# Routing per chunk inside the recurrence, a region of rows per expert, and tokens kept in expert order

## The chip, the cores and the metric

The kernel runs on one core of a Trainium2 chip. Times are device microseconds (us) of one execution. The core has five engines that run side by side, each with its own instruction stream: PE (TensorE, matrix products, with its weight loads as PEld), DVE (VectorE), ACT (ScalarE), POOL (GpSimd) and SP (SyncE, which issues transfers here). They are kept in step by semaphores that instructions raise and wait for. Transfers (DMA) can be issued by SP, ACT and POOL; an indirect one, whose rows go to addresses held in a tile, by POOL.

## What is computed

A delta-rule recurrence over 768 tokens for 4 sequences of 8 heads (head size 48), then a top-1 mixture of 8 experts, then a dense mixture of 4 experts whose shares are an input:

```python
for t in range(S):                                   # recurrence
    y[:, :, t] = q_t @ state
    state = state + bt * outer(k_t, v_t - state @ k_t)
# x = y as [3072 tokens, 384]
logits = x @ w_gate;  e_idx = argmax(logits, axis=1)  # MoE1, 8 experts, F = 1024
out[mask] = gate_w * sigmoid(x @ w_output_gate)[e] * (relu(x[mask] @ w1[e]) @ w2[e])
p = domain_probs / (domain_probs.sum(-1) + 1e-9)      # MoE2, 4 experts, F = 1024
out = sum_e p[:, e:e+1] * (relu(x @ w1[e]) @ w2[e])
```

## The kernel before, in words

**Recurrence** (to about 340 us). The 768 steps are cut into 12 chunks (NC) of 64. Each chunk needs the inverse of a triangular matrix per head, which is made in levels: DVE substitutes the small blocks (`substitute`, L1083/L1086), and PE and DVE join them over two levels; DVE turns the half-made inverse with the transpose of L1123 into X (X32), and PE multiplies with it in `level32_left` (L525). The work of chunks c+1 to c+4 is interleaved by hand in one loop over c on every engine. A chunk gives two tiles of 128 tokens (NP = 2, in all NT = 24): ACT copies them from PSUM to `x_all` (L890), PE turns them and multiplies with the gate weights, and ACT copies the logits of the chunk (L907). SP zeroes a DRAM buffer `x_sorted` (33 x 192 KB) in the meantime (`clear`).

**Routing** (340 to 390 us). With all logits there, DVE finds each token's expert (L1235 to L1241), PE sums ones below each token (its rank) and over each tile, and DVE makes of them the position of every token in an order by expert (L1246 to L1262), each expert starting at a multiple of 128 rows. POOL scatters the 24 tiles by one indirect DMA each (L480) into `x_sorted`. DVE makes a table of which expert a slot of 128 rows belongs to (`slot_i`), then the gate scale and the shares of each token. The weights of expert 0 are loaded, rounded by ACT (L986) and their low parts taken by DVE (L1298).

**MoE1** (390 to 700 us). Every product is made as three products of high and low parts (`three`: L735, L736, L737). A loop over 31 slots of 128 rows; in one pass PE does `up(s)`, turns the next tile (`tokens_turned`, L742), `down(s - 1)` and turns the hidden rows (L766). DVE takes the relu, the turned tiles (L1308, L1310) and hidden rows (L1323, L1325), and copies the result to `y_sb` (L1329). SP loads a tile ahead (`load_tile`) and writes `y_sb` to `y_sorted`. PE and ACT read a slot's expert from `slot_i` by register loads (L746, L749). POOL takes the low parts of the next expert's weights.

**Between the layers** (700 to 717 us). POOL gathers every token's row back from `y_sorted` (L501), ACT scales it (L995), PE turns it, ACT and DVE take high and low part, and POOL, ACT and DVE prepare the first half expert of MoE2.

**MoE2** (from 717 us). 4 experts in 2 halves each, over 8 blocks of 384 tokens: 64 steps of the same length. DVE adds each result, times its share, to `acc`, which is the storage of `x_all` (L1372). SP writes the tiles out (L440).

## Time and profile before

| | us |
|---|---|
| median of 3 executions | 1530.92 (1529.55 to 1543.22) |
| profiled execution, device time | 1532.9 |
| its span, first to last instruction | 1531.1 |
| PE busy | 1421.6 (93% of the span) |
| DVE busy | 664.8 (43%) |
| ACT busy | 289.8 (19%) |
| POOL busy | 256.1 (17%) |
| mean granted clock of PE | 0.96 of full speed |

Shares of busy time are averages over all stages. The granted clock is 1.00 at 2.4 GHz and 0.50 at 1.2 GHz; a stretch between shows that both occurred in it. The device time of an execution is a little above its span.

### The profile page before, as it was taken

The numbers are of one execution on the slowest core, as the hardware profiler recorded it, in microseconds if no ns is written. First come the engines' busy times: TensorE is split into PE (matmuls) and PEld (weight loads), VectorE is DVE, ScalarE is ACT, GpSimd is POOL, SyncE is SP. The second block draws the span as 40 slices with busy tenths as digits, with TensorE's granted clock in tenths as the row PEclk, the third lists the DMA queues.
The fourth block names the chain that finished last, engine by engine and source line by source line (L and its number), as shares of the span: only waits on it lengthen the run. The fifth ranks groups of instructions, "written<-read, shape, count | busy, mean of one in ns | idle before, by whom it ended". The sixth has DMA issues, their size and how long they took to land.

```text
span 1531.1 us, 36843 instructions
## 1 busy us (share of the span) xinstructions
PE 1421.6 (93%) x14814; PEld 1370.9 (90%) x14815; DVE 664.8 (43%) x1301; ACT 289.8 (19%) x631; POOL 256.1 (17%) x132
## 2 busy tenths in 40 slices
PE   5799999980799999995999999999999999999998
PEld 5799999970688888995999999999999999999998
DVE  5567676624455555553443333333333333333332
ACT  2223323122011121002331111111111111111111
POOL 1001011006533343202232002020020020200000
PEclk7899999985899999997999999999999999999999
DMA  6455454216333333114121001000010010000122
GB/s 135 99 123 125 110 119 101 73 47 249 129 113 128 123 123 121 42 42 145 47 68 42 0 0 41 0 13 28 0 41 0 0 41 0 0 0 0 28 50 46
DMA packets 106538, 99.27 MB, mean 65 GB/s; under 512 B 58128, under 2 KB 95376, under 8 KB 106448
## 3 DMA queue, kind: packets, MB, share of 16 engines
q1 hardware_dynamic: 88176, 61.81, 15.6%
q10 hardware_dynamic: 15200, 26.68, 5.4%
q0 software_dynamic: 3072, 9.44, 1.8%
q8 instruction: 75, 1.23, 0.3%
q14 instruction: 15, 0.12, 0.0%
HBM read 72.72 MB, written 25.17 MB: 64 GB/s over the span
## 4 chain that ended last, share of the span: by engine, by line
PE 84%; DMA 5%; SPq 3%; DVE 2%; POOL 2%; issue 2%; ACT 1%; ACTq 0%; DVEq 0%
PE bank L735 23%; PE bank L737 23%; PE bank L736 23%; PE bank L525 8%; DMA kq_sb<-in_kq_dram 2%; POOL x_sorted L480 2%; PE bank L766 2%; SPq L328 1%; DMA inverse_blocks<-inverse 1%; PE bank L640 1%; PE bank L643 1%; PE bank L659 1%; SPq L310 1%; PE bank L742 1%; ACT R L862 1%
## 5 line engine op out<-in xcount | busy, mean ns | idle before, releaser
L735 PE MATMUL bank<-x2Th,v1h 128*128 (+1 forms) x768 | 257.3, 335 | 3.6 <-issue 3.6
L1363 DVE SCALAR_TENSOR_TENSOR gTl<-bank,gTh 128x384 fp32r<-128x384 f32 x256 | 142.7, 557 | 269.9 <-ACT gTh L1006 269.9
L735 PE MATMUL bank<-v2h,gTh 128*128 128x384 f32 x768 | 258.3, 336 | 0.0
L737 PE MATMUL bank<-x2Th,v1l 128*128 (+1 forms) x768 | 257.1, 335 | 0.0
L736 PE MATMUL bank<-x2Tl,v1h 128*128 (+1 forms) x768 | 257.1, 335 | 0.0
L737 PE MATMUL bank<-v2h,gTl 128*128 128x384 f32 x768 | 256.6, 334 | 0.0
L736 PE MATMUL bank<-v2l,gTh 128*128 128x384 f32 x768 | 256.6, 334 | 0.0
L1006 ACT ACTIVATE gTh<-bank 128x384 fp32r<-128x384 f32 x256 | 126.0, 492 | 637.2 <-PE bank L737 637.2
L1372 DVE SCALAR_TENSOR_TENSOR x_all<-bank,p_sb,x_all 128x384 f32 (+1 forms) x192 | 106.7, 611 | 258.9 <-PE bank L737 258.9
L735 PEld LDWEIGHTS bank<-x2Th,v1h 128*128 128x128 f32 x768 | 144.7, 188 | 4.0 <-issue 4.0
L736 PEld LDWEIGHTS bank<-x2Tl,v1h 128*128 128x128 f32 x768 | 144.8, 188 | 0.0
L737 PEld LDWEIGHTS bank<-x2Th,v1l 128*128 128x128 f32 x768 | 144.6, 188 | 0.0
L736 PEld LDWEIGHTS bank<-v2l,gTh 128*128 128x128 f32 x768 | 144.3, 188 | 0.0
L735 PEld LDWEIGHTS bank<-v2h,gTh 128*128 128x128 f32 x768 | 144.3, 188 | 0.0
L737 PEld LDWEIGHTS bank<-v2h,gTl 128*128 128x128 f32 x768 | 144.2, 188 | 0.0
L510 POOL CAST v1h<-v_raw 128x1536 fp32r<-128x1536 f32 x7 | 10.3, 1473 | 478.2 <-PE bank L737 478.2
L735 PE MATMUL bank<-w2h,hTh 128*128 x248 | 86.3, 348 | 2.5 <-DVE hTl L1325 2.5
L737 PE MATMUL bank<-w2h,hTl 128*128 x248 | 84.1, 339 | 0.0
L736 PE MATMUL bank<-w2l,hTh 128*128 x248 | 83.9, 338 | 0.0
L735 PE MATMUL bank<-w1h,xsTh 128*128 x186 | 76.9, 413 | 7.5 <-issue 4.8
L525 PE MATMUL bank<-kq_sb 64*64 64x64 f32 (+1 forms) x1536 | 60.0, 233 | 16.6 <-ACT R L862 7.6
L737 PE MATMUL bank<-w1h,xsTl 128*128 x186 | 74.1, 398 | 0.0
(167 smaller groups left out, 1920.8 us busy)
## 6 DMA issues: line engine op xcount, KB each, us to landing
w_raw<-in_moe_w_dram ACTq DMA_DIRECT2D x16, 1536.0 KB, 7.0
v_raw<-in_moe_w_dram SPq DMA_DIRECT2D x16, 768.0 KB, 4.5
x_sorted<-zeros SPq DMA_DIRECT2D x33, 192.0 KB, 3.8
xs_in<-x_sorted SPq DMA_DIRECT2D x33, 192.0 KB, 2.3
y_sorted<-y_sb SPq DMA_DIRECT2D x31, 192.0 KB, 1.9
kq_sb<-in_kq_dram SPq DMA_DIRECT2D x28, 192.0 KB, 3.8
kt_sb<-in_kt_dram SPq DMA_DIRECT2D x24, 196.0 KB, 3.4
vt_sb<-in_vt_dram SPq DMA_DIRECT2D x24, 192.0 KB, 4.3
```

Source lines behind the costliest of these rows:

```text
L310: sp.dma_start(gram_blocks[n % 2, u].rearrange("h j i -> j h i"), R[rows, n % NR, :, cols])\
L328: sp.dma_start(Y[rows, n % NY, :, cols], inverse_blocks[n % 2, u].rearrange("h j i -> j h i"))\
L480: pool.indirect_dma_start(out=x_sorted, out_offset=bass.IndirectOffsetOnAxis(ap=pos[:, t:t + 1], axis=0), in_=x_all[:, t, :], in_offset=No ...
L525: return pe.matmul(dst, lhsT, rhs, start=True, stop=True)
L640: pe.matmul(bank[5 + p][half_rows(a), small(p, h)], kq_sb[half_rows(a), c % NKQ, 1, h], state[half_rows(a), c % 2, h], start=True, stop=False)
L735: pe.matmul(dst, lh, rh, start=first, stop=False)
L736: pe.matmul(dst, lh, rl, start=False, stop=False)
L737: return pe.matmul(dst, ll, rh, start=False, stop=last)
L766: ins = pe.transpose(bank[2 + half][:, 128 * m:128 * m + 128], h_sb[:, k0:k0 + 128], ident)
L1006: act.activation(gTh[:, f, :], bank[f][:, 0:BN], ACT.Relu).then_inc(g_hi, 1)
L1363: dve.scalar_tensor_tensor(out=gTl[:, f, :], in0=bank[f][:, 0:BN], scalar=0.0, in1=gTh[:, f, :].bitcast(f32), op0=ALU.max, op1=ALU.subtract)\
L1372: dve.scalar_tensor_tensor(out=a, in0=bank[4 + t][:, 0:DM], scalar=p_sb[:, bass.ds(tile, 1), bass.ds(e, 1)].rearrange("p o d -> p (o d)"), ...
```

## The change

Tokens now stay in one order, by expert, from the first layer to the output.

- Each expert has a region of 3072 + 256 rows in a DRAM buffer `x_rows`; a row holds the 384 values of a token, its logits, its key (the expert), its four shares and its number (408 values). The shares' input has a column more, the token's number.
- Two chunks behind, inside the loop, DVE finds the experts of a chunk's 256 tokens (`expert_chosen`), PE their rank within the expert (`ranks`, two products with columns for the tokens before), DVE the row (`position_taken`), and POOL sends the two tiles out (`rows_out`). Tiles stand in `rows_st`, three chunks deep.
- An expert's rows are not padded to a multiple of 128. A pass takes 128 rows from a table `pass_i`, which may begin before or end behind its expert's rows. Those are zero: 128 in front of a region (`front_rows`, from a zeroed `y_all`, in the recurrence) and 128 behind its last row (`tail_rows`, SP 4 and ACT 4, once the counts are known).
- MoE1's results are added to `y_all` at the place that `pass_i` names, so a tile at the border of two experts is summed from two passes; the extra columns are added likewise to `aux_all`. `y_sorted`, its writes and the gather are gone. 31 passes, as before.
- Expert 0's weights are loaded in chunks 9 and 10 by SP; ACT rounds w1 at the start of chunk 10; POOL takes both low parts.
- The gate scale of all tokens is made behind the relus of the last pass. The first half expert of MoE2 is loaded by ACT when expert 6 is done, and prepared by POOL. PE ends with `up(30)`, `down(29)`, `hidden_turned(30)`, the first three token tiles, `down(30)`, and goes on with MoE2.
- MoE2's first step for a block writes `acc` in place of adding to a zeroed one. POOL scatters the output by the tokens' numbers.
- The normalized shares are made in chunk 0.

```diff
-    assert NZ * (NC - 1) == NSL
+    NPASS = (N + 127) // 128 + NE - 1
...
-    x_sorted = nc.dram_tensor("x_sorted", [NSL * 128, DM], f32).ap()
-    y_sorted = nc.dram_tensor("y_sorted", [NSLOT * 128, DM], f32).ap()
...
+        def tail_rows(eng, e):
+            row = eng.value_load(tail_i[0:1, e:e + 1], min_val=REG * e + 128, max_val=REG * e + 128 + N)
+            eng.dma_start(x_rows[bass.ds(row, 128), :], y_all[:, 0:2].rearrange("p t d -> p (t d)")[:, 0:RW])\
+               .then_inc(tail_zero, 16)
...
-            def clear(c, i):
-                if c < NC - 1:
-                    s0 = 128 * (NZ * c + i)
-                    sp.dma_start(x_sorted[s0:s0 + 128, :], zeros[:]).then_inc(zero_out, 16)
...
-            def load_tile(s):
-                rows = x_sorted[128 * s:128 * s + 128, :] if isinstance(s, int) else x_sorted[bass.ds(s * 128, 128), :]
-                sp.dma_start(xs_in[:], rows).then_inc(xs_load, 16)
-
...
+            def load_rows(s):
+                row = sp.value_load(pass_i[0:1, 3, s:s + 1] if isinstance(s, int) else pass_i[0:1, 3, bass.ds(s, 1)],
+                                    min_val=0, max_val=NE * REG - 128)
+                sp.dma_start(xs_in[:], x_rows[bass.ds(row, 128), :]).then_inc(xs_load, 16)
...
+            def shares_taken(c):
+                pool.wait_ge(p_ok, 1)
+                if c >= NST:
+                    pool.wait_ge(scattered, 16 * NP * (c - NST + 1))
+                pool.tensor_copy(rows_st[:, c % NST, :, AUX + 1:AUX + 2 + E2], p_sb[:, NP * c:NP * c + NP, :]).then_inc(shares_ok, 1)
+
+            def rows_out(c):
+                pool.wait_ge(pos_ok, c + 1)
+                pool.wait_ge(shares_ok, c + 1)
+                for p in range(NP):
+                    t = NP * c + p
+                    pool.indirect_dma_start(out=x_rows, out_offset=bass.IndirectOffsetOnAxis(ap=pos[:, t:t + 1], axis=0),
+                                            in_=rows_st[:, c % NST, p, :], in_offset=None).then_inc(scattered, 16)
...
-            for t in range(NT):
-                pool.indirect_dma_start(out=x_sorted, out_offset=bass.IndirectOffsetOnAxis(ap=pos[:, t:t + 1], axis=0),
-                                        in_=x_all[:, t, :], in_offset=None).then_inc(scattered, 16)
...
+                if c == 1:
+                    pool.memset(y_all[:], 0.0).then_inc(y_zero, 1)
+                if c == NC - 1:
+                    pool.wait_ge(z32_mm, NC)
+                    low_part(w_raw1[:], w1h[:, 0], w1l[:, 0], w1_hi, w1_split, 1)
+                shares_taken(c)
+                if c >= 2:
+                    rows_out(c - 2)
+            rows_out(NC - 2)
+            rows_out(NC - 1)
+            low_part(w_raw2[:], w2h[:, 0], w2l[:, 0], w2_hi, w_ready, 1)
             for e in range(1, NE):
                 low_part(w_raw1[:], w1h[:, e % 2], w1l[:, e % 2], w1_hi, w1_split, e + 1)
...
-            def token_gather(t):
-                if t >= NXG:
-                    pool.wait_ge(xg_ok, t - NXG + 1)
-                pool.indirect_dma_start(out=xg[:, t % NXG, :], out_offset=None, in_=y_sorted,
-                                        in_offset=bass.IndirectOffsetOnAxis(ap=pos[:, t:t + 1], axis=0))\
...
+            half_expert(0)
+            pool.wait_ge(up_mm, 2 * NPASS)
             for j in range(1, 2 * E2):
                 half_expert(j)
...
+            def ranks(c, b, col):
+                pe.wait_ge(ranked_ok, 1)
+                pe.wait_ge(hot_ok, c + 1)
+                dst = bank[b][:, col:col + NP * NE]
+                pe.matmul(dst, strict_r[:], hot[:, c % 2].rearrange("p t e -> p (t e)"), start=True, stop=False)
+                pe.matmul(dst, ones_r[:], seen[:, c % 2].rearrange("p t e -> p (t e)"), start=False, stop=True).then_inc(rank_mm, 1)
+
+            def counts():
+                last = (NC - 1) % 2
+                pe.matmul(bank[2][:, 0:NE], ones_r[:], seen[:, last, NP - 1], start=True, stop=False)
+                pe.matmul(bank[2][:, 0:NE], ones_r[:], hot[:, last, NP - 1], start=False, stop=True).then_inc(count_mm, 1)
...
             gates_turned(NC - 1)
+            ranks(NC - 2, 0, 0)
...
-            pe.wait_ge(onehot_ok, 1)
-            mul(bank[0][:, 0:NT * NE], strict_up, gate_small[:, 2].rearrange("p t e -> p (t e)"))
-            mul(bank[1][:, 0:NT * NE], ones[:], gate_small[:, 2].rearrange("p t e -> p (t e)")).then_inc(rank_mm, 1)
+            ranks(NC - 1, 1, 0)
+            counts()
+            keep_warm(36)
...
                 pe.wait_ge(hT_lo, 2 * s + 2)
+                pe.wait_ge(w_ready, need)
+                pe.wait_ge(y_ok, s + 1)
...
-            with pe.Fori(1, NSLOT) as s:
+            with pe.Fori(1, NPASS - 1) as s:
                 up(s)
                 tokens_turned(s + 1)
-                pe.wait_ge(y_ok, s)
                 down(s - 1)
                 hidden_turned(s)
-            pe.wait_ge(y_ok, NSLOT)
-            down(NSLOT - 1)
-
+            up(NPASS - 1)
+            down(NPASS - 2)
+            hidden_turned(NPASS - 1)
...
+            def first_expert_up():
+                act.wait_ge(w1_in, 16 * W1_PIECES)
+                act.wait_ge(s_mm, 2 * (NC - 2))
+                act.copy(w1h[:, 0], w_raw1[:]).then_inc(w1_hi, 1)
...
+            def expert_chosen(c):
+                dve.wait_ge(lg_ok, c + 1)
+                dve.wait_ge(cleared, 3)
+                row = rows_st[:, c % NST]
+                kmax = row[:, :, AUX:AUX + 1].rearrange("p t o -> p (t o)")
+                top, equal, key = chosen[:, 0], choice[:, 0], choice[:, 1]
+                link(dve.tensor_reduce(top, row[:, :, DM:DM + NE], AX.X, ALU.max))
+                link(dve.tensor_tensor(equal, row[:, :, DM:DM + NE], over_experts(top, NP), ALU.is_equal))
+                link(dve.tensor_tensor(key, equal, over_tiles(key_row[:], NP), ALU.mult))
+                link(dve.tensor_reduce(kmax, key, AX.X, ALU.max))
+                if c:
+                    dve.tensor_tensor(seen[:, c % 2, 0], seen[:, (c - 1) % 2, 1].bitcast(f32), hot[:, (c - 1) % 2, 1].bitcast(f32), ALU.add)
+                else:
+                    dve.memset(seen[:, 0, 0].bitcast(f32), 0.0)
+                link(dve.tensor_tensor(hot[:, c % 2], key, over_experts(kmax, NP), ALU.is_equal))
+                dve.tensor_tensor(seen[:, c % 2, 1], seen[:, c % 2, 0].bitcast(f32), hot[:, c % 2, 0].bitcast(f32), ALU.add)\
+                   .then_inc(hot_ok, 1)
...
+            def position_taken(c, b, col):
+                kmax = rows_st[:, c % NST, :, AUX:AUX + 1].rearrange("p t o -> p (t o)")
+                rank = bank[b][:, col:col + NP * NE].rearrange("p (t e) -> p t e", e=NE)
+                dve.wait_ge(rank_mm, c + 1)
+                dve.tensor_tensor(choice[:, 2], rank, hot[:, c % 2].bitcast(f32), ALU.mult).then_inc(rank_read, 1)
+                dve.wait_ge(rank_read, c + 1)
+                link(dve.tensor_reduce(chosen[:, 1], choice[:, 2], AX.X, ALU.add))
+                link(dve.scalar_tensor_tensor(out=chosen[:, 2], in0=kmax, scalar=-float(REG), in1=chosen[:, 1],
+                                              op0=ALU.mult, op1=ALU.add))
+                dve.tensor_scalar(pos[:, NP * c:NP * c + NP], chosen[:, 2], float(NE * REG + 128), None, ALU.add)\
+                   .then_inc(pos_ok, 1)
...
+            def pass_tile(s):
+                return dve.value_load(pass_i[0:1, 2, s:s + 1] if isinstance(s, int) else pass_i[0:1, 2, bass.ds(s, 1)],
+                                      min_val=0, max_val=NT)
...
+                dve.tensor_tensor(xsTl[:], src, xsTh[:].bitcast(f32), ALU.subtract).then_inc(xsT_lo, 1)
+                tile = pass_tile(s)
+                aux = aux_all[:, bass.ds(tile, 1), :].rearrange("p o d -> p (o d)")
+                dve.tensor_tensor(aux, aux, xs_in[:, DM:RW], ALU.add).then_inc(aux_ok, 1)
...
+            def y_taken(s):
+                tile = pass_tile(s)
+                y = y_all[:, bass.ds(tile, 1), :].rearrange("p o d -> p (o d)")
+                dve.wait_ge(y_mm, s + 2)
+                dve.tensor_tensor(y, y, bank[4][:, 0:DM], ALU.add).then_inc(y_ok, 1)
```

The order of the instructions on three engines. On DVE, one turn of the chunk loop (chunk c = 5): `state` is the update of the state, `norms<-k_sq` the squares of a later chunk, `terms` and `inverse` the substitution. Before:

```order
L1153 TENSOR_TENSOR state<-state,bank 128x384 [waits s_mm] x2
L1032 TENSOR_REDUCE norms<-k_sq 128x16 [waits sq_ok]
L1083 TENSOR_TENSOR terms<-inverse,gram 128x2 [waits inverse_out,gram_in1]
L1086 TENSOR_REDUCE inverse<-terms 128x2 [waits sub_chain]
L1083 TENSOR_TENSOR terms<-inverse,gram 128x8 [waits sub_chain]
```

The same place of the changed kernel:

```order
L1245 TENSOR_TENSOR state<-state,bank 128x384 [waits s_mm] x2
L1278 TENSOR_REDUCE chosen<-rows_st 128x2 [waits cleared,lg_ok]
L1279 TENSOR_TENSOR choice<-rows_st,chosen 128x16 [waits rchain]
L1280 TENSOR_TENSOR choice<-choice,key_row 128x16 [waits rchain]
L1281 TENSOR_REDUCE rows_st<-choice 128x2 [waits rchain]
L1283 TENSOR_TENSOR seen<-seen,hot 128x8 [waits rchain]
L1286 TENSOR_TENSOR hot<-choice,rows_st 128x16
L1287 TENSOR_TENSOR seen<-seen,hot 128x8 [waits rchain]
L1124 TENSOR_REDUCE norms<-k_sq 128x16 [waits sq_ok]
L1175 TENSOR_TENSOR terms<-inverse,gram 128x2 [waits inverse_out,gram_in0]
```

Seven operations stand between the state and the squares. Further on in the same turn, before and then after, around the query mask `PT`:

```order
L1086 TENSOR_REDUCE inverse<-terms 128x2x5 [waits sub_chain]
L1065 TENSOR_TENSOR PT<-bank,const_sb 128x512 [waits p_mm,sub_chain]
L1083 TENSOR_TENSOR terms<-inverse,gram 128x72
L1086 TENSOR_REDUCE inverse<-terms 128x2x6 [waits sub_chain]
L1083 TENSOR_TENSOR terms<-inverse,gram 128x98 [waits sub_chain]
```

```order
L1178 TENSOR_REDUCE inverse<-terms 128x2x5 [waits sub_chain]
L1294 TENSOR_TENSOR choice<-bank,hot 128x16 [waits rank_mm,sub_chain]
L1296 TENSOR_REDUCE chosen<-choice 128x2 [waits rank_read]
L1297 SCALAR_TENSOR_TENSOR chosen<-rows_st,chosen 128x2 [waits rchain]
L1299 TENSOR_SCALAR pos<-chosen 128x2 [waits rchain]
L1157 TENSOR_TENSOR PT<-bank,const_sb 128x512 [waits p_mm]
L1175 TENSOR_TENSOR terms<-inverse,gram 128x72
L1178 TENSOR_REDUCE inverse<-terms 128x2x6 [waits sub_chain]
```

The four operations of the position stand ahead of `PT` and the rest of the substitution. On POOL, from the last chunk of the recurrence on (`vt_sb` are the values, `w1l` and `w2l` the low parts of expert 0), before:

```order
L465 TENSOR_TENSOR vt_sb<-vt_sb,length 128x768 [waits length_ok,vt_in2]
L480 DMA x_sorted<-x_all,pos 4224x384 [waits zero_out,pos_ok]
L480 DMA x_sorted<-x_all,pos 4224x384 x23
L486 MEMSET x_all 128x3072 [waits scattered]
L486 MEMSET x_all 128x3072 x2
```

and after, from the last values on:

```order
L514 TENSOR_TENSOR vt_sb<-vt_sb,length 128x768 [waits length_ok,vt_in2]
L521 COPY rows_st<-p_sb 128x2x5 [waits scattered,p_ok]
L528 DMA x_rows<-rows_st,pos 26624x408 [waits shares_ok,pos_ok]
L528 DMA x_rows<-rows_st,pos 26624x408
...
L533 TENSOR_TENSOR w1l<-w_raw_106,w1h 128x3072 [waits w1_hi,z32_mm]
L521 COPY rows_st<-p_sb 128x2x5 [waits scattered,p_ok]
L528 DMA x_rows<-rows_st,pos 26624x408 [waits shares_ok,pos_ok]
L528 DMA x_rows<-rows_st,pos 26624x408
L528 DMA x_rows<-rows_st,pos 26624x408 [waits shares_ok,pos_ok]
```

The 24 scatters in a row have become pairs, of which three (chunks 9, 10 and 11) stand behind the low part of w1. On PE, the end of the recurrence as it is now (before, the last two rows of the gates were followed by two wide products of the routing and the turning of `xs_in`):

```order
L727 MATMUL bank<-hot,strict_r 128x16 [waits hot_ok,ranked_ok]
L728 MATMUL bank<-seen,ones_r 128x16
L719 MATMUL bank<-xT_gate,wg 16x256 [waits rank_read,lg_ok,xt_ok]
L719 MATMUL bank<-xT_gate,wg 16x256 x2
L738 MATMUL bank<-const_sb,logits_T 128x16 [waits lt_ok]
...
L732 MATMUL bank<-seen,ones_r 128x8
L733 MATMUL bank<-hot,ones_r 128x8
L584 MATMUL bank<-ones 128x128 x36
L815 MATMUL bank<-const_sb,xs_in 128x128 [waits xs_load,slots_ok]
```

The ranks of chunk 10 stand ahead of the last gate product, and 36 products that only keep PE busy ahead of the first tile.

## Rows read from the trace of the kernel before

**Rows 1.** Windows by stage: length, busy time of each engine, clock, DMA share, GB/s

```profile
core 0: us, PE busy (x) PEld busy (x) DVE busy (x) ACT busy (x) POOL busy (x), PEclk, DMA share, GB/s
64.00:340.00 276.00, 265.47 (x7711) 247.90 (x7708) 176.28 (x402) 75.71 (x246) 24.45 (x20) 0.97 0.41 94
340.00:390.00 50.00, 2.52 (x7) 1.65 (x7) 20.87 (x53) 12.80 (x7) 32.10 (x26) 0.51 0.62 225
390.00:700.50 310.50, 301.75 (x1643) 273.22 (x1643) 168.68 (x279) 32.62 (x12) 98.48 (x16) 0.99 0.30 100
700.50:716.60 16.10, 2.55 (x10) 1.63 (x10) 5.30 (x10) 6.38 (x10) 6.68 (x7) 0.57 0.59 198
```

**Rows 2.** Chain of waits, 340 to 400: start us, us, what

```profile
349.24 1.25 POOL x_sorted L480
350.79 0.97 POOL x_sorted L480
...
382.93 2.56 DMA x_sorted<-x_all,pos
...
390.04 0.79 PE bank L735
```

**Rows 3.** Timeline of DVE from 339: start, us, instruction [idle before, releaser]

```profile
339.98 0.35 DVE L1235 TENSOR_REDUCE gate_tok<-logits 128x24 f32<-128x192 f32 x1 [10.87 <-ACT logits L907]
...
349.45 0.40 DVE L1270 TENSOR_TENSOR slot_cmp<-slot_cmp,expert_row 128x231 f32<-128x231 f32 x1
```

**Rows 4.** Chain of waits, 690 to 720

```profile
704.66 6.15 DMA xg<-y_sorted,pos
...
717.28 0.32 PE bank L736
```

**Rows 5.** Timelines of DVE and POOL in chunks 1 and 2 of the recurrence

```profile
95.13 0.25 DVE L1083 TENSOR_TENSOR terms<-inverse,gram 128x50 f32<-128x50 f32 x1
...
119.12 0.18 DVE L1083 TENSOR_TENSOR terms<-inverse,gram 128x18 f32<-128x18 f32 x1
...
119.85 1.47 POOL L465 TENSOR_TENSOR vt_sb<-vt_sb,length 128x768 f32<-128x768 f32 x1 [22.24 <-DMA vt_sb<-in_vt_dram]
...
120.02 1.40 DVE L1083 TENSOR_TENSOR terms<-inverse,gram 128x50 f32<-128x50 f32 x1
```

**Rows 6.** Timeline of DVE in a pass of MoE1

```profile
437.37 0.56 DVE L1329 COPY y_sb<-bank 128x384 f32<-128x384 f32 x1 [2.77 <-PE bank L737]
```

**Rows 7.** Timelines of POOL, ACT, SP, PE and DVE where expert 2's weights follow

```profile
447.05 6.81 POOL L491 TENSOR_TENSOR w2l<-w_raw,w2h 128x3072 fp32r<-128x3072 f32 x1
...
447.12 0.38 ACTq L964 DMA_DIRECT2D w_raw<-in_moe_w_dram  x1
...
447.64 0.35 SPq L417 DMA_DIRECT2D y_sorted<-y_sb  x1
...
451.71 0.49 PE L742 MATMUL bank<-const_sb,xs_in 128*128 128x128 f32 x3
...
454.72 1.29 DVE L1315 TENSOR_SCALAR h_sb<-bank 128x512 f32<-128x512 f32 x2 [4.61 <-DMA y_sorted<-y_sb]
...
458.29 0.49 PE L735 MATMUL bank<-w1h,xsTh 128*128 x1 [1.02 <-issue]
```

**Rows 8.** Instructions on `slot_i`: count, ns min/median/max, first and last start

```profile
L746 PEldq TENSOR_LOAD <-slot_i x62: 295/302/652, 388.7 to 691.8; - x62
```

**Rows 9.** Timeline, DVE's transpose and PE's product with it, chunks 2 and 9

```profile
126.21 0.71 DVE L1123 STREAM_TRANSPOSE X<-Y 128x512 f32<-128x512 f32 x1
127.72 1.49 PE L525 MATMUL bank<-X,R 64*64 64x32 f32 x45
...
293.90 0.71 DVE L1123 STREAM_TRANSPOSE X<-Y 128x512 f32<-128x512 f32 x1
295.23 1.96 PE L525 MATMUL bank<-X,R 64*64 64x32 f32 x62
```

**Rows 10.** Timeline of PE after a wait in chunk 0

```profile
76.88 2.56 PE L525 MATMUL bank<-X,R 64*64 64x32 f32 x64 [2.10 <-DVE X L1123]
```

520 lines of the change are left out of this document (295 added, 225 removed).

## The prediction

> **What bounds the kernel now.** I read the busy time by stage first, because the average over the span mixes stages with different limits. [rows 1] gives the length of each stretch and how long TensorE (PE) worked in it. In the recurrence (64 to 340 us) and the first mixture-of-experts layer (390 to 700.5) PE is busy for 96 and 97% of the time, and the second layer is like them: nothing is to be had there, but much to be lost. In 340 to 390 PE works 2.52 of 50 us, in 700.5 to 716.6 it works 2.55 of 16.1. These two gaps are what the change can win.
>
> The chain of waits names what fills them. In the first, 24 scatters stand end to end on POOL (GpSimd), the first at 349.24; the last lands from 382.93 on for 2.56, a load and the transposes follow, and the first matmul of the layer starts at 390.04 [rows 2]. The global routing on DVE (VectorE) begins at 339.98, with the last logits [rows 3]; I call that T0. In the second gap the last result is written and all tokens are gathered, 6.15 us for the first transfer alone, then scaled and turned; the first matmuls behind it take 0.32 us each [rows 4]: the granted clock is then at the lower of its two levels (1.2 GHz), after PE had been idle; ten of them cost 1.5 us.
>
> Last I looked at what stands beside POOL's long subtractions, since the change puts new DVE work there. [rows 5] shows it: a DVE product of 50 elements took 0.25 us at 95.13, and 1.40 at 120.02, where a POOL product had started 0.17 before it; DVE ended 0.1 after POOL. Both read two operands in SBUF.
>
> **Gap A.** Before: T0 to the first matmul, 390.04 - 339.98 = 50.1 us. After, from T0: six small linked operations for the expert, 0.22 each (0.18 and the link, by the row of 18 elements in [rows 5]), 1.3; two rank matmuls and semaphores 0.5 (an estimate; nothing and 1.3 are its ends); four for the position, 0.8. That is 2.6. Two scatters of 1.25 and 0.97 with 0.3 issue ahead of each end at 5.5 and land 2.56 later, at 8.1. Beside it DVE makes the pass table: two operations of 840 elements at 1.0, two of 384 at 0.56 (the copy of [rows 6]), one of 217 at 0.4 [rows 3], some 20 small ones: 7.7 us, so alone it would stand at 10.4. But from 5.5 on POOL subtracts for w2l, 6.81 us [rows 7], and DVE's next operation with two operands in SBUF is held to 12.3; what is behind it is 4.9: 17.2. The tail rows (1.67 MB, issued from 3.6 on, at the 225 GB/s of this stretch [rows 1]) land at 11.0 and don't decide. Then a register load 0.3 [rows 8], the row load with its issue 2.5, transposes and split 2.3: **22.3**. Gap A gives 50.1 - 22.3 = **27.8 us** (33.5 without the hold).
>
> **Gap B.** Removed: 16.1 us [rows 1], and the 1.5 us behind it. Against it: DVE's gate chain lies between the relus of pass 30 and hidden(30). Alone it takes 5 us, beside down(29), 4.2 us of PE; POOL's casts and low parts of the next half expert stand beside it and hold it once or twice, 1.2. So down(30) starts 1.5 later behind up(30) than now: **16.1 us**.
>
> **The recurrence.** Per chunk from c = 2 on, eleven operations on DVE: seven between the state update and the next squares, four after the fifth substitution. At 0.21, less 0.1 for each of two without link, 2.1 us. Behind them on DVE stands the transpose of X (X32), for which PE waits. In [rows 9] it ends at 126.92 in c = 2, PE starts at 127.72; less 0.06 for the semaphore the slack is 0.74. There are eight such hand-offs, c = 2 to 9, the first and the last shown; the slacks are 0.74, 0.38, 0.43, 0.38, 1.43, 1.41, 0.62, 0.56, and DVE idles another 0.29 and 0.66 ahead of it in c = 6 and 7. Beyond slack and idle time: 1.36 + 1.72 + 1.67 + 1.72 + 0.38 + 0.03 + 1.48 + 1.54 = 9.9. In c = 6 and 7 POOL's product of the values now meets a DVE product, as in [rows 5]: +2. The rank matmuls of c = 10 and 11, 0.5; PE's wait for the choices of chunks 9 and 10, 1.6; shares and constants in c = 0, 1.5; the cast of w1 on ACT at the start of c = 10 delays the gates by about 1. Together **16.5**. A wait may also bring the clock down: in [rows 10] PE idled 2.10 us and 64 matmuls took 2.56 where 62 take 1.96 in [rows 9], with what follows 1.6 us lost; a wait of 0.74 near 242 us brought none. Six waits are 1.4 to 1.7 long; I take two or three drops, **+4**, between 0 and 13.
>
> **The passes.** A pass adds on DVE two register loads and an addition of 24 columns, 0.8 together, against 2.77 idle ahead of the copy of y [rows 6]. The addition has two operands in SBUF. When an expert ends, POOL takes two low parts in a row; the first ends at 447.1 [rows 7], 9.7 us after the pass that set it off, and the addition, due at 444.3, is held to there. The row load, which now waits for the addition, is then issued at 447.9, just behind 1.5 MB of weights (447.12). What that means a row shows: the write of y of 447.64 had not landed before 454.72, when DVE went on [rows 7]; DVE's wait cost PE 1.02 us, and as much at four other experts, some 4.8 in all. Those waits go (no y is written). But the row load lands at 454.7 too, and PE is to turn the tile at 451.7 [rows 7]: 3.0 us, at the same five places 15. After half of these the clock drops, 1.6 as above: 4. With 3 for the low parts and weights of experts 1 and 2, whose phase I can't tell: 15 + 4 + 3 - 4.8, **+17**, between -5 and 25.
>
> The second layer has the same operations. At the end three scatters stand for six direct writes, with an issue and a landing in both: 0.
>
> **Sum.** 1531.1 - 27.8 - 16.1 + 16.5 + 4 + 17 = 1524.7 of span. The profiled execution took 1532.9, +1.8, and stood 2.0 above the median of 1530.92: **1524 us**, 0.4% less: within what can't be told from no change.
>
> **A rule weighed.** The rows have POOL's scatter at 349.24 for 1.25 us, and in it a DVE operation with two operands in SBUF at 349.45, which took 0.40 [rows 3] like the one before it: not held, so I cost the 20 scatters inside the recurrence at nothing. The Trainium skill, page "SBUF — State Buffer", section "SBUF: two separate sides", says that the two engines share a port pair as an exclusive lock for the whole instruction of whoever starts first, also where DVE has two SBUF inputs and POOL's instruction reads SBUF. By this rule the hold of [rows 5] was to be expected, and the trace agrees; taken for the scatters too it would add up to 20 x 0.96 = 19 us, and the trace disagrees there.
>
> **Rivals.** *The recurrence hides the work* (0.15): DVE is busy for 176 of 276 us [rows 1]; 16.5 and 4 shrink to 1: 1505. Against it: hand-offs with 0.4 to 1.4 for 2.1.
> *Holds and queue don't bite* (0.17): the addition slips in before POOL, or the loads don't queue behind the weights; w2l comes late. The passes lose 1 or gain up to 5, gap A gives 33.5: 17 + 5.7 less, 1502. For it: the rows have a write behind the weights, no read.
> *POOL keeps the port* (0.15), which ends slower than before: its two low parts are back to back [rows 7], and if DVE isn't let in between, the addition waits another 6.8 us, hidden(s) with it, 5.4 us of PE, and the row load meets the second 1.5 MB, 3.8 more: 9.2 x 5 = 46 in place of 15, 1555. It decides from 4.4 us a place above what is in the sum already, 22 in all. For it: nothing shows a turn between two such products. Against: the only product held ended right behind POOL's.
> *The recurrence loses more* (0.12): a drop at each of eight waits, 9 more, and scatters that hold DVE for half of 19: 1543.
> That the change does nothing is excluded: scatters and gather leave the gaps. The forecast itself, 1512 to 1536, keeps 0.41, a tenth of it below 1515.6.
>
> **Numbers.** 1% is 15.3 us, about what a measurement of this kernel tells from no change. Faster (below 1515.6): 0.15 + 0.17 + 0.04 = 0.36; same 0.37 of the forecast and half of the fourth, 0.43; slower (above 1546.2) 0.15 and the other half, 0.21. The range is 1500 to 1550, from the second rival to past the fourth; the third is left out.
>
> **What would show it.** Right: the first matmul of the layer 22 us after the last logits, with a DVE product of 7 us beside w2l; the turn to the second layer without a gap above 5 us; hand-offs without slack in c = 2 to 9 and a recurrence 17 to 22 us longer; PE waits of about 3 us at five experts' ends, each behind an addition held by POOL. Wrong: slack in the hand-offs, additions of 0.2 throughout, or ones of 10 us.

## The result

The changed kernel takes 1577.28 us (median of 4 runs, 1575.25 to 1583.23), the kernel before 1532.39 beside it (4 runs). The ratio is 1.029, with an interval of 1.023 to 1.035: **slower by 2.9%**, where 1524 us and a range of 1500 to 1550 were predicted. The profiled execution took 1583.23 us, with a span of 1581.3, and lies 6 us above the median; the span before was 1531.1.

Both traces are cut at the same three events: T0, the end of the last logits; the first matmul of MoE1; the first matmul behind the turn to the second layer.

| stretch | before | after | difference | predicted |
|---|---|---|---|---|
| start to T0 (recurrence) | 339.98 | 387.22 | +47.2 | +20.5 |
| T0 to first matmul of MoE1 (gap A) | 50.06 | 22.96 | -27.1 | -27.8 |
| MoE1 and the turn (gap B within) | 326.59 | 357.03 | +30.4 | +0.9 |
| the rest | 814.47 | 814.09 | -0.4 | 0 |
| span | 1531.1 | 1581.3 | +50.2 | -6.4 |

So gap A came out to 0.7 us, and two stretches missed, by 26.7 and 29.5 us. Busy time by stage in the changed kernel, the columns as in [rows 1]:

```profile
64.00:387.20 323.20, 297.56 (x7758) 271.95 (x7755) 199.49 (x528) 79.84 (x253) 61.77 (x56) 0.89 0.37 90
387.20:410.20 23.00, 11.25 (x80) 10.72 (x80) 16.98 (x38) 2.64 (x1) 9.55 (x4) 0.79 0.36 125
410.20:767.20 357.00, 321.69 (x1649) 287.79 (x1650) 208.97 (x323) 44.65 (x26) 114.67 (x22) 0.92 0.28 92
```

In the recurrence PE works 297.6 of 323.2 us, where it worked 265.5 of 276 [rows 1]. 32 more microseconds of work for 47 matmuls more is not more work: the granted clock fell from 0.97 to 0.89. As an estimate, 0.11 of 323 us less 0.03 of 276 us makes some 27 of the 32. The other 15 are waits. In MoE1 with the turn PE is busy for 321.7 us instead of 304.3 (the last two rows of [rows 1] together), at a clock of 0.92, and waits 13 us longer.

**What PE waits for in the recurrence.** The new rank product (L727) needs the choices of the experts, which DVE makes behind the state update. The chain of waits alone misleads here: it goes from the end of the state's 64 products at 215.53 over DVE's choices (216.03 to 218.39) to L727 at 218.53, as if PE stood idle for 3.0 us. PE's own timeline of the same turn (c = 5) shows that it does not:

```profile
213.44 2.07 PE L584 MATMUL bank<-delta,kt_sb 64*64 64x48 f32 x64
215.34 2.02 PE L584 MATMUL bank<-X,R 64*64 64x32 f32 x64
217.20 1.13 PE L584 MATMUL bank<-kq_sb 64*64 64x64 f32 x32
218.53 0.25 PE L727 MATMUL bank<-hot,strict_r 128*128 128x16 f32 x1 [0.20 <-DVE seen L1287]
...
221.34 0.29 PE L702 MATMUL bank<-delta,PT 64*64 64x48 f32 x3 [0.43 <-issue]
222.09 0.24 PE L702 MATMUL bank<-delta,PT 64*64 64x48 f32 x1 [0.46 <-issue]
...
222.37 3.16 PE L584 MATMUL bank<-Y,Z 64*64 64x32 f32 x64
```

96 other products stand between, and PE waits 0.20 us for the choices. It pauses twice more for 0.4 us, for nothing that the trace shows, and then 64 products take 3.16 us where those at 215.34 took 2.02. PE's waits from 64 to 387 us (us in total, times, longest):

```profile
PE bank L584 <- DVE X L1215: 9.3, 3, 5.4
PE bank L727 <- DVE seen L1287: 3.5, 7, 1.1
```

The waits for the choices are 3.5 us in the whole recurrence; in the turns c = 2 to 9 none is longer than 0.45. The pauses that nothing releases make 8.1 us in 19 pieces, for 1.6 before. The longest wait of all is at the hand-off of X (from DVE's transpose to PE) in turn c = 2:

```profile
139.71 3.62 PE L584 MATMUL bank<-X,R 64*64 64x32 f32 x64 [5.40 <-DVE X L1215]
```

There POOL's memset of `y_all` (127.15 to 135.25) holds the last operation of the positions, and what stands behind it on DVE, until 135.3. Two stretches from one hand-off of X to the next, first before, then after, the columns as in [rows 1]:

```profile
76.83:101.34 24.51, 23.49 (x666) 22.10 (x668) 16.89 (x42) 7.04 (x24) 2.44 (x2) 0.93 0.59 133
126.92:151.47 24.55, 24.21 (x738) 22.77 (x736) 17.88 (x43) 7.66 (x26) 2.36 (x2) 1.00 0.54 128
```
```profile
79.17:107.65 28.48, 28.42 (x684) 27.21 (x686) 16.81 (x43) 7.11 (x24) 2.51 (x3) 0.76 0.39 84
139.66:172.32 32.66, 31.40 (x720) 29.59 (x720) 18.30 (x53) 7.68 (x26) 4.65 (x5) 0.77 0.33 81
```

The first follows a wait of 3.41 us (2.10 before), the second the wait of 5.40. In both PE hardly waits any more; it is slow, at a clock of 0.76 and 0.77, and the stretches are 4.0 and 8.1 us longer than before. By these hand-offs the recurrence is late by 2.3, 6.3, 12.7 and 20.9 us in c = 0 to 3; the other 26 come in steps of 2 to 6 us, c = 4 to 10. In c = 5 DVE's hand-off even has slack, as the instructions on `X` from 226 to 232 us show (duration in ns, first and last start):

```profile
L584 PE MATMUL bank<-X,R x44: 205/219/219, 230.8 to 232.0; 64*64 64x32 f32 x44
L1215 DVE STREAM_TRANSPOSE X<-Y x1: 711/711/711, 226.5 to 226.5; 128x512 f32<-128x512 f32 x1
```

DVE has X at 227.2 and PE takes it at 230.8; before, in [rows 9], PE took it 0.80 us after its end. Behind slow products PE is late, not DVE.

**Gap A.** Timelines of DVE and POOL behind T0, and PE's first matmul of the layer, changed kernel:

```profile
387.22 0.17 DVE L1278 TENSOR_REDUCE chosen<-rows_st 128x2 f32<-128x16 f32 x1 [1.58 <-ACT rows_st L993]
...
391.79 7.28 DVE L1389 TENSOR_TENSOR by_expert<-by_expert 128x8 f32<-128x8 f32 x1
392.35 6.68 POOL L533 TENSOR_TENSOR w2l<-w_raw,w2h 128x3072 fp32r<-128x3072 f32 x1
...
410.18 0.79 PE L808 MATMUL bank<-w1h,xsTh 128*128 x1 [1.33 <-DVE xsTl L1421]
```

The product of 8 elements held for 7.28 us by the 6.68 us subtraction is the one predicted: it was to end 12.3 us behind T0 and ends 11.85 behind it. The first matmul stands at 22.96 for a predicted 22.3.

**The passes.** The chain of waits where expert 0's passes end (changed kernel):

```profile
479.28 5.96 DMA xs_in<-x_rows
...
485.83 1.30 issue
```

and the timelines of POOL, DVE, ACT's queue and PE there:

```profile
471.50 6.84 POOL L533 TENSOR_TENSOR w1l<-w_raw,w1h 128x3072 fp32r<-128x3072 f32 x1 [40.66 <-ACT w1h L1075]
475.70 2.69 DVE L1424 TENSOR_TENSOR aux_all<-aux_all,xs_in 128x24 f32 x1 [0.29 <-issue]
...
478.37 0.37 ACTq L1057 DMA_DIRECT2D w_raw<-in_moe_w_dram  x1
...
485.28 0.55 PE L815 MATMUL bank<-const_sb,xs_in 128*128 128x128 f32 x3 [2.08 <-DMA xs_in<-x_rows]
487.30 0.18 DVE L1424 TENSOR_TENSOR aux_all<-aux_all,xs_in 128x24 f32 x1 [0.28 <-issue]
```

Each step of the mechanism is there as it was written. The addition comes at 475.70 while POOL subtracts (471.50 to 478.34), ends with it at 478.39, the weights are issued at 478.37, the row load stands behind them, takes 5.96 us, and PE waits 2.08 for it. The next pass's addition takes 0.18. But the loss is larger than the wait: another 1.30 idle before the first product, and products of 0.32 instead of 0.17 for some time.

**Gap B.** DVE and POOL at the turn (timelines, changed kernel):

```profile
741.80 0.34 DVE L1464 TENSOR_REDUCE gate_tok<-aux_all 128x24 f32<-128x192 f32 x1
...
745.28 3.48 POOL L533 TENSOR_TENSOR v1l<-v_raw,v1h 128x1536 fp32r<-128x1536 f32 x1
745.45 3.35 DVE L1468 CAST id_i<-aux_all 128x24 int32<-128x24 f32 x1
...
750.25 3.42 POOL L533 TENSOR_TENSOR v2l<-v_raw,v2h 128x1536 fp32r<-128x1536 f32 x1
750.29 3.41 DVE L1472 TENSOR_SCALAR gate_tok<-gate_tok 128x24 f32<-128x24 f32 x1
...
756.53 0.18 DVE L1478 TENSOR_TENSOR scale_tok<-gate_tok 128x24 f32<-128x24 f32 x1
```

The gate chain takes 14.9 us (741.80 to 756.71) for a predicted 6.2: the cast waits for POOL's v1l, L1472 for its v2l, and two products of 192 elements at 742.18 and 743.79, ahead of them, took 1.69 and 1.62 beside the end of POOL's low part before and its cast. Four operations are held.

### The profile page after: what moved, and what is told of

Read it like the earlier page. It is cut to its first block, busy times and chain, and to the rows that moved or that the text cites. A ratio compares the mean times of both kernels' runs of the same rounds, so it can differ in the third digit from the quotient of the medians.

```text
span 1581.3 us, 37643 instructions
## 1 busy us (share of the span) xinstructions
PE 1471.8 (93%) x14905; PEld 1409.0 (89%) x14906; DVE 720.9 (46%) x1449; ACT 287.6 (18%) x629; POOL 278.6 (18%) x151
## 3 DMA queue, kind: packets, MB, share of 16 engines
q0 software_dynamic: 3072, 9.74, 1.7%
HBM read 68.00 MB, written 16.22 MB: 53 GB/s over the span
## 4 chain that ended last, share of the span: by engine, by line
PE 81%; DVE 8%; DMA 5%; issue 3%; SPq 1%; ACT 1%; DVEq 0%; another core or an unknown queue 0%; POOL 0%; ACTq 0%; POOLq 0%
PE bank L808 22%; PE bank L809 21%; PE bank L810 21%; PE bank L584 10%; DMA xs_in<-x_rows 3%; PE bank L842 1%; PE bank L699 1%; PE bank L719 1%; PE bank L702 1%; DVE aux_all L1424 1%; ACT R L945 1%; PE bank L815 1%; DMA kq_sb<-in_kq_dram 1%; DVE terms L1175 1%; SPq L380 1%
## 5 line engine op out<-in xcount | busy, mean ns | idle before, releaser
L810 PE MATMUL bank<-x2T,v1l 128*128 (+1 forms) x768 | 256.5, 334 | 0.0
L808 PE MATMUL bank<-x2T,v1h 128*128 (+1 forms) x768 | 256.5, 334 | 0.0
L809 PE MATMUL bank<-x2T,v1h 128*128 (+1 forms) x768 | 256.5, 334 | 0.0
L1507 DVE SCALAR_TENSOR_TENSOR y_all<-bank,aux_all,y_all 128x384 f32 x168 | 96.3, 615 | 244.7 <-PE bank L810 244.7
L809 PEld LDWEIGHTS bank<-x2T,v1h 128*128 128x128 f32 x768 | 144.2, 188 | 0.0
L808 PEld LDWEIGHTS bank<-x2T,v1h 128*128 128x128 f32 x768 | 144.2, 188 | 0.0
L810 PEld LDWEIGHTS bank<-x2T,v1l 128*128 128x128 f32 x768 | 144.2, 188 | 0.0
L808 PE MATMUL bank<-w2h,hTh 128*128 x248 | 93.0, 375 | 7.5 <-issue 6.4
L533 POOL TENSOR_TENSOR w1l<-w_raw,w1h 128x3072 fp32r<-128x3072 f32 x8 | 54.5, 6814 | 220.1 <-ACT w1h L1075 213.0
L809 PE MATMUL bank<-w2l,hTh 128*128 x248 | 89.9, 362 | 0.0
L810 PE MATMUL bank<-w2h,hTl 128*128 x248 | 89.3, 360 | 0.0
```

The source lines that it names most:

```text
L533: pool.tensor_tensor(lo, raw, hi.bitcast(f32), ALU.subtract).then_inc(lo_ok, 1)
L808: pe.matmul(dst, lh, rh, start=first, stop=False)
L809: pe.matmul(dst, lh, rl, start=False, stop=False)
L810: return pe.matmul(dst, ll, rh, start=False, stop=last)
L1507: dve.scalar_tensor_tensor(out=a, in0=bank[4 + t][:, 0:DM], scalar=share, in1=a, op0=ALU.mult, op1=ALU.add).then_inc(acc_ok, 1)
```

## The experiments

Four theories stood after this. **R**: in the recurrence PE's wait for the choices (its place in PE's order) is what costs. **D**: DVE's added work ahead of X costs, wherever the ranks stand. **Q**: the row loads behind the weights cost the passes far more than 15 us. **S**: POOL's holds of DVE at the turn and in gap A cost. The kernels ran in four groups, each on one chip with its own runs of the kernel before (medians 1534.64, 1534.37, 1536.65 and 1535.12 us). The table gives the same cuts as above for all of them; MoE1 is with the turn, the rest is 814.1 to 814.2 in every one. T0, gap A, MoE1 and the span are of the profiled execution, the median of all executions.

| kernel, chip | T0 | gap A | MoE1 | span | median us | ratio to before |
|---|---|---|---|---|---|---|
| e_ranks, 1 | 367.17 | 23.06 | 356.39 | 1560.8 | 1560.46 | 1.016 (1.010 to 1.022) |
| e_idle, 1 | 349.96 | 22.96 | 357.01 | 1544.1 | 1548.03 | 1.010 (1.004 to 1.016) |
| e_tiles, 1 | 386.51 | 22.72 | 317.29 | 1540.7 | 1535.82 | 0.999 (0.997 to 1.002) |
| e_all, 1 | 361.98 | 16.22 | 309.94 | 1502.3 | 1499.51 | 0.976 (0.970 to 0.982) |
| e_best, 2 | 352.03 | 16.39 | 308.69 | 1491.2 | 1494.01 | 0.973 (0.969 to 0.977) |
| e_memset, 2 | 383.09 | 23.18 | 351.81 | 1572.2 | 1574.08 | one execution |
| e_reduce, 2 | 379.08 | 22.91 | 323.93 | 1540.1 | 1541.97 | one execution |
| e_copy, 2 | 376.53 | 22.93 | 368.67 | 1582.3 | 1584.16 | one execution |
| e_shares, 3 | 366.33 | 16.17 | 310.30 | 1506.9 | 1507.95 | 0.981 (0.979 to 0.983) |
| e_nowarm, 3 | 371.52 | 16.51 | 309.85 | 1512.0 | 1516.67 | 0.987 (0.986 to 0.989) |
| e_gate, 3 | 395.46 | 22.90 | 349.46 | 1581.9 | 1583.86 | one execution |
| e_table, 3 | 379.82 | 16.65 | 354.50 | 1565.1 | 1567.02 | one execution |
| e_deep3, 4 | 348.28 | 16.19 | 311.60 | 1490.2 | 1489.53 | 0.970 (0.968 to 0.972) |
| e_best3, 4 | 348.74 | 16.22 | 310.06 | 1489.1 | 1489.68 | 0.971 (0.968 to 0.974) |
| e_nowarm3, 4 | 347.45 | 16.41 | 309.53 | 1487.5 | 1487.18 | 0.969 (0.965 to 0.974) |

One thing is needed to read it. The recurrence of one and the same code differs between executions: in the changed kernel, and in e_tiles, e_copy, e_reduce, e_table and e_gate, which leave it as it is, T0 is 387.2, 386.5, 376.5, 379.1, 379.8 and 395.5. So a difference in T0 between chips says nothing below about 10 us, and on one chip a profiled execution can lie several us from the median (e_tiles 6.8 above it); gap A repeats to half a microsecond, and MoE1 with the turn, where its code is the changed kernel's, is 351.8 to 357.0.

**e_ranks: the ranks later in PE's order.** The two rank matmuls stand behind everything else of the chunk, and with them DVE's positions:

```
# PE, chunk c
-                if c >= 2:
-                    ranks(c - 2, 7, 320)
                 read_out(c, 0)
...
                     level32_right(c + 1)
+                if c >= 2:
+                    pe.wait_ge(lg_ok, c)
+                    ranks(c - 2, 7, 320)
...
# DVE, chunk c
-                if c >= 2:
-                    position_taken(c - 2, 7, 320)
                 if ahead:
                     query_masked(c + 3, 0)
...
                 if onward:
                     level32_taken(c + 1)
+                if c >= 2:
+                    position_taken(c - 2, 7, 320)
```

> The changed kernel with one thing moved: PE makes the ranks of chunk c-2 at the end of its turn c (behind level32_right) and no longer ahead of read_out(c,0); DVE takes the position at the end of its turn too. The choice of the expert stays where it was on DVE, and all work is the same. Theory 1 (PE waits some 3 us per chunk for the choice, and the clock falls behind each wait): the recurrence, 387.2 us to the last logits in the changed kernel and 340.0 before, shortens by 20 to 27 us, the rest stays, time about 1552. Theory 2 (the loss comes from the two microseconds of DVE work ahead of the transpose X, and from scatters beside DVE): it shortens by at most 6 us, time 1571 or more.

T0 came at 367.17, 19.3 us earlier than in e_tiles, which ran on the same chip with the recurrence of the changed kernel. That is near the 20 to 27 us of Theory 1, but the edit does not separate R from D: with the two matmuls, the four operations of the position go behind the transpose of X, and the memset's hold of them with it. PE's waits, e_tiles first (64 to 387 us), then e_ranks (64 to 367 us):

```profile
PE bank L589 <- DVE X L1220: 12.4, 8, 5.4
...
PE bank L732 <- DVE seen L1292: 3.2, 6, 1.1
```
```profile
PE bank L584 <- DVE X L1217: 6.8, 5, 3.6
```

The waits for X fell by 5.6 us, those for the choices had been 3.2 in all. 9.3 of the 19.3 us are gained between the hand-offs of c = 1 and c = 3 (61.9 us in e_tiles, 52.6 here), where the memset's hold stood ahead of X. So D has a part in this gain, and what the place of the ranks in PE's order is worth by itself was not tested; a kernel with the ranks moved and the positions left in place would tell. What is left is 27 us over before.

**e_idle: the choices in DVE's idle time as well.** On top of e_ranks, `expert_chosen(c - 2)` moves behind the key lengths, where DVE waits for PE anyway:

```
-                if c >= 2:
-                    expert_chosen(c - 2)
                 if c + 4 < NC:
                     squares_summed(c + 4)
...
                     key_lengths(c + 4)
+                if c >= 2:
+                    expert_chosen(c - 2)
```

> As the run with the ranks moved, and the choice of the expert on DVE is moved too, from behind the state update to behind the key lengths, where DVE waits for PE anyway. Theory 1 (PE's wait for the ranks is the loss): no more than 4 us below the run with the ranks alone. Theory 2 (DVE work ahead of X): here the recurrence shortens by another 10 us or more. By either, what is left is the memset of y_all on POOL in chunk 1 (about 8 us), the wait for w1 in chunk 10 (6) and the shares in chunk 0 (2), so 355 us to the last logits and a time of about 1545.

T0 349.96: another 17.2 us. This edit takes seven more DVE operations from ahead of X. PE's waits for X (64 to 350 us) are down to the one of turn c = 0:

```profile
PE bank L584 <- DVE X L1217: 3.2, 1, 3.2
```

D holds: with both edits all eleven added operations stand behind X, and 36.5 of the 46.5 us by which e_tiles stood over before are gone. PE's busy time between 64 us and T0 goes from 298.9 over 288.5 to 273.9 us, at a clock of 0.87, 0.90 and 0.95, so most of the gain is the clock that comes back and not the waits themselves. The medians, less what differs in gap A and MoE1, give some 15 and 13 us for the two steps instead of 19.3 and 17.2 (an estimate). The remaining 10 are in the chunks that neither touches, below.

**e_tiles: the row load cut in two.** The 384 values of the row are loaded as soon as PE has turned the last tile, the 24 others alone wait for the addition:

```
-                sp.dma_start(xs_in[:], x_rows[bass.ds(row, 128), :]).then_inc(xs_load, 16)
+                sp.dma_start(xs_in[:, 0:DM], x_rows[bass.ds(row, 128), 0:DM]).then_inc(xs_load, 16)
...
+                # behind a wait for aux_ok
+                sp.dma_start(aux_in[:], x_rows[bass.ds(row, 128), DM:RW]).then_inc(aux_load, 16)
```

> The changed kernel, but the row load of a pass is two transfers: the 384 values go out as soon as PE has turned the tile before, and only the 24 extra columns, to a tile of their own, wait for DVE's addition. Theory 1 (an addition held by POOL for 2.7 us sends the row load out behind 1.5 MB of weights, PE waits 3 us, and the clock falls for 3 more): the pairs of passes of 12.0 and 13.3 us at five experts go back to 9.6, MoE1 shortens by 30 to 38 us, time about 1543. Theory 2 (DVE itself is late, through register loads and the held addition): at most 10 us, time 1567 or more.

MoE1 fell from 357.0 to 317.3 us, **39.7 less**, and stood at 356.4 and 357.0 in e_ranks and e_idle, of its chip. The addition is still held as it was (2.67, 0.18, 0.18, 2.67 in consecutive passes), but nothing that PE needs stands behind it. Q holds: it is the load's place behind 1.5 MB, not the held addition, that costs.

**e_all** puts e_idle, e_tiles, the early y memset, the gate chain and the pass table free of POOL, and the cast of w1 at the end of chunk 10 together. **e_best** is e_all without the early memset, on another chip.

> Both moves in the recurrence and the split row load together, and four more: the memset of y_all at the start of the program; the cast of w1 at the end of chunk 10 on ACT; POOL's low part of w2 of expert 0 behind the pass table; POOL's half expert 1 behind the gate scale. If the causes are the ones named and independent, recurrence 345 us to the last logits (47 longer becomes 5), gap A 17 us (23 before), MoE1 as long as in the kernel before, turn to the second layer 6 us shorter than in the changed kernel: time about 1490, below the kernel before. If the loss is spread work rather than waits, 1530 or more.

> As the run with all six edits, but the memset of y_all goes back from the start of the program to chunk 1. In the run with all six a DVE operation of 16 elements took 7.45 us beside that memset at the start, and every later hand-off stood 5 to 6 us later than in the run with the two moves alone. If that is the cause, the last logits come at 350 to 356 us and the time is 1491 to 1496. If something else among the edits (the later cast of w1) lengthened the recurrence by 12 us, the last logits stay at 362 and the time at 1500.

e_all is 2.4% (1.8 to 3.0) and e_best 2.7% (2.3 to 3.1) faster than the kernel before, so both beat the change and what it replaced. Gap A is 16.2 and 16.4 us, MoE1 309.9 and 308.7: the turn and the layer together are 17 and 18 us shorter than before. T0 came at 361.98 in e_all, for the 345 expected: on one chip its recurrence is 12 us *longer* than e_idle's, from which it differs there by the memset and the cast only. 6 of the 12 are there at the hand-off of c = 0, behind the early memset; the other 6 come in c = 6, where PE waits 2.29 us for ACT's `logits_T` and the clock drops. In e_best T0 is 352.03, inside the 350 to 356 expected, though on another chip. In e_best a held addition (426.08, 2.67 us) and the next (435.57, 0.18 us) stand 9.49 us apart, the period of an undisturbed pass.

**e_memset: the early memset alone.** `pool.memset(y_all[:], 0.0)` goes from chunk 1 to the start of the program, ahead of POOL's first values. It takes 8.10 us, and in the changed kernel it meets the first positions:

```
+            pool.memset(y_all[:], 0.0).then_inc(y_zero, 1)
             values(0)
...
-                if c == 1:
-                    pool.memset(y_all[:], 0.0).then_inc(y_zero, 1)
```

> The changed kernel with one thing moved: the memset of y_all on POOL from chunk 1 to the start of the program. Theory 1 (a memset on POOL holds DVE's operations with one small SBUF operand and one SBUF result, but not products and reductions): chunks 1 and 2 shorten by 5 us (the position of chunk 0, held for 5.1 us, goes free), the start lengthens by 5 to 6, the time stays within 3 us of 1577. Theory 2 (a memset holds nothing, and the 5.1 us had another cause): nothing changes in either place.

The changed kernel first, then e_memset, timelines of POOL and DVE:

```profile
127.15 8.10 POOL L546 MEMSET y_all<- 128x9600 f32 x1
...
129.01 0.24 DVE L1175 TENSOR_TENSOR terms<-inverse,gram 128x50 f32<-128x50 f32 x1
...
130.14 5.13 DVE L1299 TENSOR_SCALAR pos<-chosen 128x2 int32<-128x2 f32 x1
```
```profile
9.92 7.45 DVE L1139 TENSOR_SCALAR length<-norms 128x16 f32<-128x16 f32 x1
...
133.11 0.17 DVE L1298 TENSOR_SCALAR pos<-chosen 128x2 int32<-128x2 f32 x1
```

The hold of 5.13 us goes and one of 7.45 comes at the start. The hand-off of chunk 2 is 5.4 us nearer to that of chunk 1 (26.6 instead of 32.0), that of chunk 0 is 3.9 later, and T0 is within the scatter of its code (383.1, for 379.1 and 376.5 in e_reduce and e_copy on the same chip). So the memset takes about 5 us where it stands, with the positions ahead of X, and 4 where I put it: no gain. It is also seen that the memset holds the two operations with a scalar, and not the product at 129.01.

**e_reduce and e_copy: what kind of DVE operation is held.** The held operation is the addition of 24 columns. Both kernels put an operation of another kind ahead of it, which alone gates the row load:

```
+                dve.tensor_reduce(extra[:], xs_in[:, DM:RW].unsqueeze(2), AX.X, ALU.add).then_inc(aux_ok, 1)   # e_reduce
+                dve.tensor_copy(extra[:], xs_in[:, DM:RW]).then_inc(aux_ok, 1)                                # e_copy
                 dve.wait_ge(aux_ok, s + 1)
                 dve.tensor_tensor(aux, aux, extra[:], ALU.add).then_inc(aux_sum, 1)
```

> The changed kernel, but the extra columns leave xs_in by a DVE reduction over an axis of one element (one operand in SBUF) into a tile of their own, which releases xs_in; the addition follows from there. Theory 1 (what is held is an operation with two operands in SBUF): the reduction takes 0.2 us everywhere, the load goes out 3 us earlier and ahead of the weights, MoE1 with the turn is 317 to 325 us long instead of 357. Theory 2 (any DVE operation is held while POOL subtracts): the reduction is held for 2.7 us as the addition was, 357 stays.

> As the run with the reduction, with a plain copy from SBUF to SBUF in its place. Theory 1 (copies, casts and operations with a scalar from SBUF to SBUF are held too, as the cast of 24 elements for 3.35 us and the addition of a constant for 3.42 us at the end of MoE1 suggest): held for 2.7 us like the addition, 357 us stays. Theory 2 (only two operands matter): 317 to 325 us like the reduction.

First e_reduce, then e_copy, POOL and DVE at an expert's end:

```profile
456.06 6.85 POOL L535 TENSOR_TENSOR w1l<-w_raw,w1h 128x3072 fp32r<-128x3072 f32 x1 [33.71 <-ACT w1h L1077]
460.08 0.18 DVE L1426 TENSOR_REDUCE extra<-xs_in 128x24 f32<-128x24 f32 x1 [0.19 <-issue]
460.40 2.54 DVE L1428 TENSOR_TENSOR aux_all<-aux_all,extra 128x24 f32 x1
```
```profile
461.46 6.86 POOL L535 TENSOR_TENSOR w1l<-w_raw,w1h 128x3072 fp32r<-128x3072 f32 x1 [41.44 <-ACT w1h L1077]
465.48 2.87 DVE L1426 COPY extra<-xs_in 128x24 f32<-128x24 f32 x1 [0.19 <-issue]
468.26 6.79 POOL L535 TENSOR_TENSOR w2l<-w_raw,w2h 128x3072 fp32r<-128x3072 f32 x1
468.49 6.60 DVE L1428 TENSOR_TENSOR aux_all<-aux_all,extra 128x24 f32 x1
```

In the same POOL subtraction the reduction takes 0.18 us, and the addition behind it is held. With the reduction MoE1 is 323.9 us, with the copy 368.7, for 351.8 in e_memset of the same chip: moving the row load's gate to an operation that isn't held gives 28 us, most of what e_tiles gives. The Trainium skill, page "SBUF — State Buffer", section "Who interferes with whom", says that a reduction of DVE never contends with GpSimd on this chip, a copy in its fast mode with any instruction of GpSimd, and an operation with two SBUF inputs with one that reads SBUF. The three rows and the two of the memset agree with each part. The copy shows something else as well. Its addition comes 0.2 us behind the start of POOL's *second* subtraction and waits for all of it, 6.60 us. In the changed kernel the addition was already waiting when the first ended, and got in between.

**e_gate and e_table: the two other holds.** In e_gate POOL begins the first half expert of the second layer when the gate chain is through; in e_table its low part of w2 waits for the pass table:

```
-            pool.wait_ge(up_mm, 2 * NPASS)
+            pool.wait_ge(scale_ok, 1)          # e_gate
...
+            pool.wait_ge(slots_ok, 1)          # e_table, ahead of the low part of w2 of expert 0
```

> The changed kernel with one wait changed: POOL prepares half expert 1 of the second layer only when the gate scale is there. Theory 1 (POOL's casts and subtractions hold DVE's gate chain, 15 us from its first operation to the scale instead of 5): half expert 0 still holds it for some 5 us, the rest goes, and MoE1 with the turn shortens by 4 to 6 us, 352. Theory 2 (the chain is long by itself): 357 stays.

> The changed kernel with one wait changed: POOL takes the low part of w2 of expert 0 only when the pass table is there. Theory 1 (it holds DVE's table for 7.3 us): the first matmul of MoE1 comes 16 to 17 us after the last logits instead of 23. Theory 2 (DVE was held by something else, or the rows in memory decide): 21 us or more.

In e_gate the gate chain takes 7.2 us (749.73 to 756.97), and MoE1 with the turn 349.5 us, 5.0 less than in e_table of the same chip. The passes in it vary too; from the addition of the last pass to the second layer's first matmul it is 23.8 us in e_gate, 31.4 in e_table and 31.1 in the changed kernel. On another chip e_all takes 7.4 us less than e_tiles for MoE1 with the turn, 7.3 of them in this last stretch. In e_table the first matmul stands 16.65 us behind T0, and 22.90 in e_gate beside it: 6.3 us, for 5.7 that the prediction gave the hold. The product that was held for 7.28 takes 0.17 there.

**The rest of the recurrence.** Starting from e_best three things were tried that might hide in the last 10 us: the shares of chunk 0 later in DVE's order (e_shares), no products that only keep PE busy ahead of the first tile (e_nowarm), a fourth buffer for the staged rows, with a semaphore for each (e_deep3). The last three kernels of the table share a chip.

```
-                if c == 0:                       # e_shares: to the end of the iteration
-                    constants_ranked()
-                    shares_normalized()
...
-            keep_warm(36)                        # e_nowarm, e_nowarm3
...
-    NST = 3                                      # e_deep3
+    NST = 4
```

> The version with five edits (e_best) and a sixth: the rounded constants and the normalized shares of chunk 0 on DVE move from behind the state update to the end of chunk 0. If they stand on the path there, as I costed them (1.5 us), the hand-off of X in chunk 1 comes 1.5 to 2.5 us earlier and the last logits with it; time 1492. If chunk 0 is bound elsewhere, no change: 1494.

> The version with five edits (e_best) without the 36 products that keep PE busy ahead of the first tile (nothing of the result depends on them). Theory 1 (they hold the clock through the start of MoE1): the first matmuls of the layer run at half clock for longer, MoE1 with the turn becomes 2 to 4 us longer, time 1496. Theory 2 (they delay the first tile): gap A becomes shorter by up to 2 us.

> The version with five edits (e_best), with rows_st four chunks deep instead of three (its scatters counted by four semaphores; two small tiles of the substitution share their place with two tiles of y_all, which are zeroed later for it). Theory 1 (ACT's copy of a tile waits for the scatter of three chunks before to land, which moves the turn of the tiles and with it the gates): the last logits come at 342 to 348 us, and the time is 1480 to 1487, at least 8 us below e_best on the same chip. Theory 2 (the landing doesn't decide): as e_best on the same chip.

> The version with five edits (e_best) once more, unchanged, on the chip of the others of this call. It ran at 0.973 of the kernel before on one chip; the version without the keep-warm products, whose recurrence is the same program, had its last logits 19 us later on another. If the chip makes that difference, this run may come anywhere from 1490 to 1515, and near to the version without the products.

> The version without the 36 keep-warm products once more, on the same chip as e_best3. If these products only matter for the clock at the start of MoE1, it stands 1 to 4 us above e_best3, with the same recurrence; if they matter for the recurrence (where they do not run), 15 us above.

On the last chip the three are alike: 1489.53, 1489.68 and 1487.18 us. Neither the fourth buffer nor the 36 products change anything that can be measured. (For the fourth buffer in the changed kernel itself, where the scatters stand closer to the next use, there is no result.) On the third chip both kernels miss what was expected: e_nowarm takes 29.5 us more than the same code, e_nowarm3, on the last chip, 24.1 of the 24.5 between the profiled spans in the recurrence, and e_shares 18 more than e_best3. The chain of waits of e_nowarm there, and then one group of PE's from 64 to 340 us (busy us, mean ns, idle time and its releasers), in e_nowarm and in the same code on the last chip, e_nowarm3:

```profile
230.24 0.42 issue
230.66 0.32 PE bank L590 x3
```
```profile
L590 PE MATMUL bank<-Y,Z 64*64 64x32 f32 x1344 | 48.1, 225 | 4.0 <-issue 3.5 <-ACT Z L976 0.5
```
```profile
L590 PE MATMUL bank<-Y,Z 64*64 64x32 f32 x1408 | 46.5, 222 | 0.9 <-ACT Z L976 0.9
```

PE pauses 0.42 us in the middle of products that wait for nothing the trace shows; 3.5 us of it in this group, none in this group on the other chip. The changed kernel's own trace has such pauses too (above), and e_tiles, with the same recurrence, has none of these short ones and the same T0. e_shares is inconclusive: its only partner on that chip has a second edit. Its hand-off of X in turn c = 0 comes 2.3 us earlier (74.44 for 76.77), as expected, and at T0 it is 5.2 ahead, but the difference in between moves from 3.1 to 0.6 us.

## Why the prediction was wrong

**What bounds the kernel, gap A, the tail: right.** The hold, its place and its length are as written; so are the scatters, the load and PE's start, to 0.7 us. The 5.7 us set for the hold do not follow from the terms as written (17.2 with the hold, and 11.0 without it, where the tail rows land, make 6.2); e_table gives 6.3.

**The step that failed: the price of a clock drop.** The prediction read it from one place, [rows 10], where a wait of 2.10 us was followed by a short slow stretch: "with what follows 1.6 us lost". It took "two or three drops, **+4**, between 0 and 13" for the recurrence and the same 1.6 for the passes. The larger part of both misses is in this term.

**Recurrence, +47.2 for +20.5.** From 64 us on, PE's idle time grew by 15.1 us, where the waits were to add 16.5, and its busy time by 32.1, where the drops were to add 4. The two stretches behind the waits of c = 0 and c = 2 ran at a clock of 0.76 and 0.77. By that, 0.24 of 28.5 us and 0.23 of 32.7 us are lost, some 7 us each (an estimate), where [rows 10] had shown 1.6. Why the clock stays down for so much longer than there stays open. The mechanism of the 9.9 us, DVE's work ahead of X, is right, and e_ranks with e_idle shows it. That the waits fit as a sum is in part luck. The longest, 5.40 us, comes from the memset of `y_all`, which the sum had at nothing and without a reason; the pauses that nothing releases (8.1 us) weren't in it either; and in this trace only 0.5 us of PE's waits for X are left after c = 2 (in e_tiles, the same order, 3.8 up to c = 9), for the 8.5 that the terms of c = 3 to 9 make. The rank products, taken as a wait of 0.5 and 1.6 us at the last chunks, cost 3.5 us of waiting in all.

About 10 us stay in e_idle, where no added operation stands ahead of X. At the hand-offs of X it is 1.0 us late in c = 0, 5.6 in c = 1, 5.2 in c = 9, 8.2 in c = 10 and 10.0 at T0. So one half comes behind the wait for X in c = 0 (3.16 us, for 2.10 before; the clock is 0.73 from there to the next hand-off, for 0.93), where the shares and constants stand, and the other half at the end. In c = 10 of the changed kernel ACT waits 10.62 us for the raw weights in its own order ahead of the gates:

```profile
349.50 2.75 ACT L1025 CAST w1h<-w_raw 128x3072 fp32r<-128x3072 f32 x1 [10.62 <-DMA w_raw<-in_moe_w_dram]
```

The sum had 1 us for the cast and nothing for its wait for the load; PE waits 2.00 us for ACT behind it. From this hand-off of X to the next there are 27.0 us, for 20.7 before.

**Passes, mechanism right, term mis-sized.** The held addition, the load behind the weights and the wait of PE are as predicted, at five places, and POOL let DVE in between its two subtractions, so the third rival did not occur. PE's wait for the load is 2.00 to 2.25 us, 10.5 at five places, for the 15 in the sum. What was mis-sized is again what follows: "After half of these the clock drops, 1.6 as above: 4". Two passes around an expert's end take 25.5 us (475.70 to 501.21 for the additions) where two undisturbed ones take 19.2. Of these 6.3 us, 2.08 are the wait, 1.30 idle time ahead of the first product, and some 2.6 are 17 products at 0.32 instead of 0.17 us. The five places lose 30.2 us together, so 20 behind the waits for the 4 of the sum. The first three passes lose another 6.3 against e_tiles (experts 1 and 2), where 3 were set. With 3.2 spread over the rest this makes the 39.7 that e_tiles gave back, for 15 + 4 + 3 = 22: **17.7 missed**.

**Gap B, the chain of it.** It was to be held "once or twice, 1.2"; it is held four times, and without POOL beside it the stretch is 7.4 us shorter: **6.2 missed**. The kind of row that would have said it is that of [rows 5] and [rows 7]: a gate chain of a dozen linked operations, most with two SBUF inputs or a scalar, beside subtractions that come one after the other. What is left of the stretch when both are taken away is e_all: 309.9 us for 326.6 before, 16.7 gained, where the sum's gains (16.1, the 4.8 of the old waits, and the 1.2) make 22.1: **5.4 missed**. Two waits of PE in e_all's trace make about as much. One is 3.96 us early in the layer, where an addition that comes 0.46 us behind the start of POOL's subtraction is held for 6.38 us, ahead of `hidden(0)`. The other is 3.4 us in two pieces at the turn, where 1.5 were allowed. Together 39.7 + 7.4 - 16.7 = 30.4, the difference measured.

**The rule weighed.** Scatters inside the recurrence hold nothing. Timelines of POOL and DVE in the changed kernel:

```profile
219.26 1.04 POOL L528 DMA_INDIRECT x_rows<-rows_st,pos  x1 [0.16 <-issue]
...
219.54 0.17 DVE L1175 TENSOR_TENSOR terms<-inverse,gram 128x8 f32<-128x8 f32 x1
```

Of some 80 DVE operations that run beside a scatter in this trace none takes 0.1 us more than its kind does elsewhere, so they were rightly costed at nothing. For POOL's arithmetic the rule held in every row shown here, and more often than the sum allowed.

**The chances.** The change ended on the slower side, which had 0.21. The rival nearest to it, "the recurrence loses more" at 1543, had the right kind of loss, more drops, but at 1.6 us each, and scatters that hold DVE, which didn't occur. The range had no room for the recurrence and the passes both missing on the same side.

## What to carry to other kernels

When work goes into a tuned loop, put it behind the hand-offs that another engine waits for: eleven operations, 2.1 us of DVE work a chunk, stood ahead of one here, and moving them behind it gave back 36.5 us. Price a wait of PE at its length plus the slower products behind it, and read that price from more than one place: it was 1.6 us behind one wait in the kernel before, and some 7 behind each of two longer ones here. Ask of every wait in a chain what the waiting engine did meanwhile, in its own timeline. Never put a small load that PE needs soon behind a large one in time: the same row load, split and issued earlier, was worth 40 us. Put short DVE operations that others wait for where GpSimd does no arithmetic, or give the gate to one that isn't held.

## What the runs showed of the hardware

- A DVE operation that waits while GpSimd works gets its turn between two GpSimd subtractions (2.69 us in all), but one that comes 0.2 us into the second waits for it whole (6.60).
- A memset of GpSimd, which reads nothing, holds DVE's operations with a scalar: one on 2 elements for 5.13 us, one on 16 for 7.45, while a product with two SBUF inputs beside the same memset takes 0.24.
- A 204 KB read issued less than 1 us behind a 1.5 MB one took 5.96 us, for a median of 2.5 over all 31.
- The recurrence of one code took between 376 and 396 us in six executions of the changed order, and between 347 and 372 in four of e_best's, while the second layer repeated to 0.1. What makes the difference stays open. Some traces, on the third chip and of the changed kernel itself, have pauses of about 0.4 us in PE that nothing releases.
